# Two expert sums ahead of a tile's Relu, and one expert's maximum between a write and its wait

## The reference, cut to what matters

```python
def _moe2_ref(x, w_gate, w_noise, noise, w1, w2):      # x 3072 x 512, 8 experts, F = 1024
    ...                                                # noisy logits, top two experts per row, weights top2_w
    for e in range(E):
        for k in range(2):
            mask = top2[:, k] == e
            h = np.maximum(x[mask] @ w1[e], 0.0)
            out[mask] += top2_w[mask, k, None] * (h @ w2[e])
```

## Time and profile before

| | |
|---|---|
| median of 3 runs | 539.69 us (538.48 to 541.95) |
| profiled execution | 539.68 us |
| its span in the trace | 537.8 us |
| PE busy | 492.4 us, 92% |
| PEld, DVE, POOL, ACT busy | 291.5, 276.2, 254.2, 185.8 us |
| mean granted TensorE clock | 0.982 |

### The profile page before, as it was taken

The page is one execution under the profiler, slowest core; times in us unless marked ns, Lnnn a source line. Parts: engine busy times, 40 slices in busy tenths (PEclk is TensorE's granted clock), DMA queues, the critical chain, the costliest instruction groups (busy, mean ns, idle before and its releaser), DMA issues.

```text
span 537.8 us, 13565 instructions
## 1 busy us (share of the span) xinstructions
PE 492.4 (92%) x4844; PEld 291.5 (54%) x4845; DVE 276.2 (51%) x443; ACT 185.8 (35%) x346; POOL 254.2 (47%) x217
## 2 busy tenths in 40 slices
PE   3999999987978667989999999999999999999995
PEld 3877787863567243444544544545545445445452
DVE  2676766666221897463646455464545332433422
ACT  0222222221003537665455363554442222223210
POOL 2222222202000024525777868786878766666553
PEclk9999999998997889999999999999999999999999
DMA  7999999989999999342466342132232332433410
GB/s 276 400 359 398 401 401 404 380 340 333 403 425 424 390 417 400 112 174 85 161 217 198 102 137 49 27 58 45 44 59 44 53 47 43 57 42 42 60 20 2
DMA packets 35096, 107.93 MB, mean 201 GB/s; under 512 B 11871, under 2 KB 13135, under 8 KB 32624
## 3 DMA queue, kind: packets, MB, share of 16 engines
q1 hardware_dynamic: 20880, 92.90, 44.6%
q0 software_dynamic: 14176, 14.49, 14.8%
HBM read 93.87 MB, written 29.43 MB: 229 GB/s over the span
## 4 chain that ended last, share of the span: by engine, by line
PE 76%; DMA 13%; DVE 3%; issue 3%; POOL 2%; ACT 1%; SPq 1%; DVEq 0%; POOLq 0%
PE ps L1019 47%; DMA w_region<-moe_w 7%; PE ps L1002 4%; PE ps L672 4%; PE ps L736 4%; DMA late_w1a<-chunks 4%; PE ps L856 3%; PE ps L885 3%; DMA out<-s_region,rec_region 2%; PE ps L712 2%; PE ps L726 2%; PE ps L747 2%; PE ps L686 1%; POOL out L625 1%; SPq L524 1%
## 5 line engine op out<-in xcount | busy, mean ns | idle before, releaser
L1019 PE MATMUL ps<-w_region,s_region 128*128 (+1 forms) x1304 | 290.4, 379 | 2.0 <-DVE s_region L1704 1.0
L1019 PEld LDWEIGHTS ps<-w_region,s_region 128*128 128x128 f16 x1304 | 125.4, 98 | 143.4 <-issue 2.8
L1674 DVE SCALAR_TENSOR_TENSOR s_region<-ps,s_region 128x1024 f16<-128x1024 f32 x55 | 67.3, 1224 | 144.2 <-ACT s_region L1232 144.1
L1232 ACT ACTIVATE s_region<-ps 128x1024 f16<-128x1024 f32 x55 | 56.3, 1024 | 176.5 <-PE ps L1002 176.5
L619 POOL DMA_INDIRECT out<-s_region,rec_region x41 | 53.9, 1315 | 49.4 <-DVE s_region L1704 46.1
L625 POOL DMA_INDIRECT out<-s_region,rec_region x42 | 66.9, 1593 | 19.2 <-issue 11.9
L613 POOL DMA_INDIRECT rec_region<-records,idx x55 | 60.1, 1092 | 24.4 <-issue 16.3
L559 POOL TENSOR_TENSOR s_region<-w_region,s_region 128x512 f32<-128x512 f32 x14 | 14.6, 1043 | 50.0 <-PE ps L747 31.9
L1002 PEld LDWEIGHTS ps<-s_region,sw_region 128*128 (+1 forms) x440 | 29.6, 98 | 14.0 <-issue 0.8
L1704 DVE TENSOR_SCALAR s_region<-ps,rec_region,y_scale 128x512 f32<-128x512 f32 x42 | 33.8, 805 | 5.9 <-PE ps L1019 4.1
L1002 PE MATMUL ps<-s_region,sw_region 128*128 128x128 f16 x440 | 34.5, 219 | 0.5 <-ACT s_region L1227 0.4
(11 more groups left out here) (249 smaller groups left out, 571.1 us busy)
## 6 DMA issues: line engine op xcount, KB each, us to landing
w_region<-moe_w SPq DMA_DIRECT2D x49, 512.0 KB, 11.2
w_region<-moe_w SPq DMA_DIRECT2D x10, 2048.0 KB, 8.7
w_region<-chunks SPq DMA_DIRECT2D x26, 512.0 KB, 7.2
s_region<-moe_w SPq DMA_DIRECT2D x4, 2048.0 KB, 12.9
sw_region<-chunks SPq DMA_DIRECT2D x12, 512.0 KB, 7.2
late_w1a<-chunks SPq DMA_DIRECT2D x8, 512.0 KB, 8.2
w_region<-moe_w SPq DMA_DIRECT2D x3, 1024.0 KB, 8.0
s_region<-moe_w SPq DMA_DIRECT2D x5, 512.0 KB, 8.4
```

Source lines behind the costliest of these rows:

```text
L1019: last = nc.tensor.matmul(bank[6 + r], h[:, r, f, :], w2b_parts[:, bass.ds(o, 1), part, f, :].rearrange("p e m -> p (e m)"), start=(first ...
L1232: nc.scalar.activation(h_hi[:, r, :, :].rearrange("p c t -> p (c t)").rearrange("p (a n) -> p a n", a=2), ps[:, 2 + 2 * r:4 + 2 * r, :], A ...
L1674: nc.vector.scalar_tensor_tensor(out=h_lo[:, r, :, :].rearrange("p c t -> p (c t)").rearrange("p (a n) -> p a n", a=2), in0=ps[:, 2 + 2 * ...
```

## The change

On ACT both sums of o = 1 stand together behind `stage_c(2)` and ahead of `keep_ct(2)` and tile 1's Relu; `keep_ct(3)` goes ahead of tile 2's Relu. On POOL the maximum of o = 1 goes ahead of fetches 6 to 10 (and so of tile 0's write), and the maximum of o = 2 between tile 2's write and the wait for tile 1's write. On DVE scale and `scale_y` of o = 1 go ahead of `low_keep(0)`, those of o = 2 to the head of tile 4, ahead of `h_low(5)` and `keep_y(4)`. The other experts stay where they were.

```diff
@@ POOL
             sw_all_sum(*SW_GROUPS[2])
-            for i in range(4, 2 * DEPTH + 3):
+            for i in range(4, DEPTH + 2):
+                fetch_records(i)
+            w2b_all_sum(EARLY)
+            for i in range(DEPTH + 2, 2 * DEPTH + 3):
                 fetch_records(i)
...
                 if i >= 1:
 
+                    if i == SUMS[EARLY + 1] - 2:
+                        w2b_all_sum(EARLY + 1)
                     pool.wait_ge(out_written[(i - 1) % DEPTH], 16 * ((i - 1) // DEPTH + 1))
                 add_rows(i)
                 if 2 * DEPTH + 3 <= i + DEPTH + 2 < RT:
                     fetch_records(i + DEPTH + 2)
-                if i == 0:
-                    w2b_all_sum(EARLY)
                 for o in FIRST:
-                    if i == SUMS[o] - 1:
+                    if o > EARLY + 1 and i == SUMS[o] - 1:
                         w2b_all_sum(o)
@@ ACT
             sw_high(7)
             sw_keep(14)
-            w2b_sum_part(EARLY, 0, junk)
             stage_c(2, 0, rec_arrival(2))
+            w2b_sums(EARLY, junk)
+            keep_ct(2, 0)
             h_high(1, 1)
-            keep_ct(2, 0)
             stage_c(3, 1, rec_arrival(3))
+            keep_ct(3, 1)
             h_high(2, 0)
-            keep_ct(3, 1)
-            w2b_sum_part(EARLY, 1, junk)
             w2b_high(EARLY)
@@ DVE
-            low_keep(0, 0, None)
-            h_low(2, 0)
             w2b_scale_by_sum(EARLY)
             dve.wait_ge(order_ready, 1)
             scale_y(EARLY)
+            low_keep(0, 0, None)
+            h_low(2, 0)
             w2b_low(EARLY)
             keep_y(1, 1, None)
             for i in range(2, UNROLLED):
+                if i == SUMS[EARLY + 1]:
+                    w2b_scale_by_sum(EARLY + 1)
+                    scale_y(EARLY + 1)
                 low_keep(i, i % DEPTH, i // DEPTH if i >= DEPTH else None)
                 for o in FIRST:
-                    if i == SUMS[o]:
+                    if o > EARLY + 1 and i == SUMS[o]:
                         w2b_scale_by_sum(o)
                         scale_y(o)
```

## The result

| | before | after |
|---|---|---|
| median of 14 runs | 539.55 us (537.85 to 542.81) | 536.17 us (535.06 to 540.1) |
| ratio | 1 | 0.9931, 95% interval 0.9911 to 0.9951 |
| profiled execution, span | 539.68, 537.8 us | 540.1, 538.3 us |

What follows compares the result with a forecast made beforehand. PE was taken to set the pace, with only 1.99 us of its waits winnable. The terms −0.99 + 0.42 − 1.00 = −1.57 us took 539.68 us to 538.1 us; the range was 537.1 to 540.3 us.

Steps and rivals of the forecast that it cites:

- (a): At out_b(3, first): register work or a larger price at hidden_b(2) eats keep_y(1)'s win; 538.7 us, chance 0.22.
- (b): At turn_c(7): POOL reaches the maximum of o = 2 too late, scale near 249 as before; 539.1 us, chance 0.08.
- (c): POOL's queue: writes pile up behind the load of o = 3, PE waits at out_b(5, not first); about 541.1 us, chance 0.08.
- the good end: POOL at the maximum of o = 2 at about 239, then waiting for ACT's second sum at 241.7; scale ready at 243.3.
- the bad end: Nothing of POOL passes from 227.4 to 232.0, beside w2b_low(1); maximum of o = 2 reached at 244.8, scale at 246.4.
- The price of the pair: At hidden_b(2): both sums ahead of keep_ct(2) make it 0.42 us late, and PE loses 0.42 in a new stall.
- the prediction's lower case: At hidden_b(2): the pair costs 0.2 us if PE's own preceding matmuls were what held it at 220.85.
- all that this change can win on PE's path is 1.99 us: PE's waits: 0.99 us at out_b(3, first) plus 1.00 us at turn_c(7), or 0.4% of the time.
- The first stall: PE's 0.99 us wait at out_b(3, first) for DVE's keep_y(1); to go whole, 0.57 us won after the pair's 0.42.
- The second stall: PE's 1.00 us wait at turn_c(7) for stage_c(7), queued on ACT behind a half awaiting its scale; to go whole.

Runs made afterwards that it cites:

- stage4_early: Kernel before, with stage_c(4) on ACT moved ahead of the second expert's high halves; stretch hidden_b(1) to hidden_b(7) 38.98 us, before 38.72.
- o1_only: The change without its o = 2 lines (maximum and scale of o = 2 in old places); stretch 37.95 us, ratio to before 1.0018.
- after_again: The changed kernel unaltered, run again as a control against the kernel before; ratio 0.9889 (0.9859 to 0.9918), stretch 35.83 us.

## Why the prediction was wrong

The direction and the mechanism of both stalls held. Both went whole, and rivals (a), (b) and (c) all fell. `keep_y(1)` was to end 14.7 us behind `hidden_b(1)` and ended 14.1 behind it. POOL reached the maximum of o = 2 in time, near the good end, where ACT's sum comes last. Of the chain in (c), tile 0's write went out at 231.33, ahead of the load of o = 3 (236.97), and `add_rows(1)` had no wait for it. The fetches beside `w2b_low(1)` weren't stretched to over 2 us, as was foretold: the write and the add behind them were (2.11 and 2.56 us), where the bad end had POOL shut out for 4.6 us.

The price of the pair came out right by luck. It was put at 0.42 us, all of it at `hidden_b(2)`, with an idle there. `keep_ct(2)` did come 0.42 us later (2.51 us behind `hidden_b(1)` for 2.09), but `hidden_b(2)` only 0.25, with no idle listed: before, it wasn't `keep_ct(2)` that held it but PE's own matmuls (219.12 and 8 of them is 220.85), which was the prediction's lower case. Another 0.19 were lost from `hidden_b(2)` to `out_b(1, first)` (1.46 us for 1.27), for which the prediction had no term.

What failed is the sentence "all that this change can win on PE's path is 1.99 us", and the two terms of the sum taken from it.

- The first stall was entered as 0.99. It measured 2.03: an idle of 0.69 named issue belonged to it, which stage4_early moved over to `keep_y(1)`, and PE's idle is counted from the end of the last matmul. A matmul of `out_b` is listed with 379 ns while the next starts 216 ns behind it (24 of them take 5.34 us), so each gap hides 0.16 us. By starts, `turn_c(4)` to the matmul behind it took 0.91 us for 0.05, and the 8 matmuls to 235.01 took 2.89 for 1.73: 0.86 + 1.16 = 2.02.
- The second stall was entered as 1.00 and measured 1.18 for the same reason. It also wasn't a constant: it hangs on the landing of tile 1's write. `add_rows(2)` waited 4.40 us for it in the profile that I read and 4.72, 4.74 and 4.96 in the three others, and tiles 6 to 7 took 6.86 against 7.04, 7.20 and 7.25. The forecast came from the mildest of four executions.
- With the right sizes my own sum would have been −2.03 + 0.44 − 1.18 − 0.12 = −2.89 us, 536.8 us, just below the stated range's lower end of 537.1. The 0.12 are tiles 4 to 6, which no term of the prediction stands for (`hidden_b(4)`, right behind the stall, is 0.57 us from `turn_c(5)` and not 0.45). The lower end should have lain near 535.5: both stalls whole (3.21), 0.4 for the late one's spread, and the 0.6 by which the prediction widened. One execution in four of before had 3.2 us more, which is in no such end.

The prediction took the parts as additive. They aren't: alone, the early part wins 1.68 us up to `hidden_b(6)`, of which 0.91 are taken back at `turn_c(7)` (o1_only), because the late stall's end is tied to a transfer more than to PE. The intervals of 0.9931 and 0.9959 overlap. The 0.9889 of after_again, on a chip where before took 544.13 us, isn't explained. The stall of 4.09 us was seen on that chip and would fit it if it came often there, but it was seen once, in an execution of 541.84 us, and that wasn't tried further.

## What to carry to other kernels

Size a stall on PE by the pitch of what repeats (here 5.68 us a tile), not by the idle that the profile lists, and look at every idle put down to issue for a semaphore wait of the sequencer just ahead of it. Two stalls in a row aren't a sum: if the later one ends by something that moves less than the engine does, it takes back part of what removing the earlier one wins, so they have to go together. And look for the idle of the helping engine (ACT's 1.2 us here) before pulling work ahead of something that PE waits for.

## What was not expected of the hardware

On POOL a transfer's instruction isn't always held by DVE's `w2b_low`: one of 2.11 and one of 2.56 us were, but the fetch that had begun at 230.03, 0.2 us before the first half did (230.21), took its usual 1.00 beside it.
